# One level of a blocked linear attention summed with tokens as rows, and a two-part activation moved between engines

## The reference

```python
f = 1.0 / (1.0 + np.exp(-f_logit))
for t in range(S):
    state = f[:, :, t, :, None] * state + np.einsum('bhd,bhe->bhde', k[:, :, t], v[:, :, t])
    y[:, :, t] = np.einsum('bhd,bhde->bhe', q[:, :, t], state)
# y as (3072, 384), then
h = x @ w_in                                   # 384 -> 2048
g = np.where(h >= 1, h, np.where(h <= -1, 0.0, (h + 1) ** 2 / 4))
x = g @ w_out                                  # 2048 -> 384
g = x @ w_gate                                 # 384 -> 1536
out = (g * sigmoid(g) * (x @ w_val)) @ w2_out  # 1536 -> 384
```

## Time and profile before the change

| what | value |
|---|---|
| median of three runs | 1029.41 us |
| profiled execution | 1029.71 us, its span 1027.9 us |
| PE busy | 995.3 us, 97% of the span |
| DVE, ACT, POOL busy | 490.3, 466.0, 428.5 us |
| share of PE in the chain that ended last | 89% |
| DMA | 63.61 MB; packets of the SP queue took 16.7% of 16 engines' span |

### The profile page before, as it was taken

How to read it: one execution, slowest core, us unless ns; L and a number is a source line. 1 busy time by engine, 2 the same in 40 slices (tenths; PEclk the granted TensorE clock), 3 DMA queues, 4 the chain that set the end, 5 groups by cost and what they waited for, 6 DMA issues and landing times.

```text
span 1027.9 us, 19928 instructions
## 1 busy us (share of the span) xinstructions
PE 995.3 (97%) x8277; PEld 829.4 (81%) x8277; DVE 490.3 (48%) x615; ACT 466.0 (45%) x851; POOL 428.5 (42%) x360
## 2 busy tenths in 40 slices
PE   4789999999999999999999999999999999999998
PEld 4678688888888888888888888888888888888886
DVE  6879848745954874594355422222222222232221
ACT  5854767657666765766355322221222222221221
POOL 7769736652763565375265222222222222222222
PEclk9989999999999999999999999999999999999999
DMA  9360134015004201300541010010100100000000
GB/s 357 124 226 2 63 99 160 1 44 185 33 2 173 86 2 46 121 32 2 185 139 47 1 62 1 6 56 1 55 7 1 62 1 1 32 0 1 31 1 32
DMA packets 17802, 63.61 MB, mean 62 GB/s; under 512 B 1968, under 2 KB 2352, under 8 KB 16944
## 3 DMA queue, kind: packets, MB, share of 16 engines
q1 hardware_dynamic: 17712, 62.33, 16.7%
HBM read 52.89 MB, written 9.44 MB: 61 GB/s over the span
## 4 chain that ended last, share of the span: by engine, by line
PE 89%; POOL 3%; issue 3%; DVE 2%; ACT 1%; DMA 1%; SPq 0%; ACTq 0%; POOLq 0%; DVEq 0%
PE acc L568 11%; PE acc L569 10%; PE acc L570 10%; PE bank L595 7%; PE bank L594 7%; PE bank L596 7%; PE hid L554 6%; PE hid L556 6%; PE hid L555 6%; PE bank L407 4%; PE hid L595 2%; PE hid L594 2%; PE hid L596 2%; PE bank L474 2%; POOL keys L1120 1%
## 5 line engine op out<-in xcount | busy, mean ns | idle before, releaser
L1162 POOL TENSOR_TENSOR g_lo<-prod,g_hi 128x512 fp32r<-128x512 f32 x72 | 93.1, 1293 | 347.7 <-ACT g_hi L846 347.7
L1155 POOL TENSOR_TENSOR g_lo<-act_tmp,g_hi 128x512 fp32r<-128x512 f32 x96 | 128.2, 1335 | 166.5 <-ACT g_hi L807 166.5
L1053 DVE TENSOR_TENSOR sig<-sig,bank 128x512 f32<-128x512 f32 x72 | 49.6, 688 | 275.4 <-ACT sig L840 275.4
L846 ACT CAST g_hi<-prod 128x512 fp32r<-128x512 f32 x72 | 44.7, 621 | 248.1 <-PE acc L570 248.1
L1120 POOL TENSOR_TENSOR keys<-keys,gates 128x512 f32<-128x512 f32 x82 | 108.1, 1319 | 71.2 <-PE bank L407 46.5
L554 PE MATMUL hid<-x_hi,win_hi 128*128 128x512 f32 (+1 forms) x291 | 116.5, 400 | 0.8 <-DVE act_tmp L1041 0.6
L568 PE MATMUL acc<-g_hi,wout_hi 128*128 128x512 f32 x288 | 114.1, 396 | 1.2 <-POOL g_lo L1155 1.2
L556 PE MATMUL hid<-x_hi,win_lo 128*128 128x512 f32 (+1 forms) x291 | 113.0, 388 | 0.0
L555 PE MATMUL hid<-x_lo,win_hi 128*128 128x512 f32 (+1 forms) x291 | 112.9, 388 | 0.0
L569 PE MATMUL acc<-g_lo,wout_hi 128*128 128x512 f32 x288 | 112.2, 390 | 0.0
L570 PE MATMUL acc<-g_hi,wout_lo 128*128 128x512 f32 x288 | 112.2, 390 | 0.0
(11 more groups left out here) (102 smaller groups left out, 1936.0 us busy)
## 6 DMA issues: line engine op xcount, KB each, us to landing
gates<-in_f_dram SPq DMA_DIRECT2D x12, 512.0 KB, 4.9
queries<-in_q_dram SPq DMA_DIRECT2D x12, 512.0 KB, 4.6
keys<-in_k_dram SPq DMA_DIRECT2D x12, 512.0 KB, 4.7
values<-in_v_tok_dram SPq DMA_DIRECT2D x6, 1024.0 KB, 7.7
q_tok<-in_q_tok_dram SPq DMA_DIRECT2D x12, 384.0 KB, 7.7
k_tok<-in_k_tok_dram SPq DMA_DIRECT2D x12, 384.0 KB, 8.2
x_dram<-x_out SPq DMA_DIRECT2D x6, 768.0 KB, 3.4
x_raw<-x_dram SPq DMA_DIRECT2D x6, 768.0 KB, 5.6
```

What stands on the lines that cost most here:

```text
L1155: pool.tensor_tensor(g_lo[:, c % RING, :], act_tmp[:, 2 + c % 2, :], g_hi[:, c % RING, :].bitcast(F32), ALU.subtract).then_inc(g_lo_done, 1)
```

## The change

Three things change.

1. From the third unit on (`APART = 2`) level 1 is no longer done by PE. The score of a token with the one before it is the sum over 48 dimensions of query times gate times the earlier key. The host lays out gates and queries shifted by one token, with tokens as rows (`f_next`, `q_next`). They are loaded into `q_tok` after its own product is summed; ACT takes the sigmoid (`next_gate`), POOL multiplies the keys by it (`next_key`), the shifted queries are loaded into the same place, DVE multiplies (`next_own`) and sums (`next_sum`) into `nexts`, and four masked copies with `nexts` as the source (`place_nexts`) put them where the two level-1 takes had put theirs. The level's `copy_right`, `level` and `take_level` go; its `scale_q` and `scale_k` stay. The four parts of `place_diag` move to other half slots, and levels 2 to 8 come one half slot earlier.
2. In the first unit the own product and sum come before the scaling of level 32, and no longer wait for POOL's keys.
3. The activation: ACT takes max((h+1)/2, 0) (`Relu`) from the bank, then squares it, and one DVE operation takes the minimum with 1 and the maximum with h. The clamp on DVE is gone.

The core of the diff ("..." where lines are left out):

```diff
-FIRST = Plan(own=(), diag=(20, 22), own_v=(21, 23), ...
+FIRST = Plan(own=(), diag=(18, 20), ... own_v=(21, 22), ...
 def usual(levels, whole, last, y, **others):
-    p = Plan(own=(-13, -12), diag=(-11, -10), own_v=(), place=(-9, -8, -6, -4), sigmoid=(-2, -1), gated=(-1, 0),
+    p = Plan(own=(-13, -12), diag=(-11, -10), own_v=(), next_gate=(-9, -8), next_key=(-8, -7), next_own=(-5, -4), next_sum=(-4, -3), next_place=(1, 2, 3, 4),
+             place=(-5, -3, 0, 1), sigmoid=(-2, -1), gated=(-1, 0),
...
-USUAL = usual((2, 5, 8, 11, 13), 16, 19, 21)
+USUAL = usual((1, 4, 7, 10, 13), 16, 19, 21, sigmoid=(-3, -2), gated=(-2, 0))
+USUAL = USUAL._replace(scale=[0, 1] + USUAL.scale[2:], turn=[0, 1] + USUAL.turn[2:])
...
+        def load_next_gates(a):
+            for g in range(2):
+                sp.wait_ge(diag_done, 2 * a + g + 1)
+                sp.dma_start(tok_group(q_tok, g), tok_group(fn[a], g)).then_inc(fn_in[g], 16)
+        def load_next_queries(a):
+            for g in range(2):
+                sp.wait_ge(next_keyed, 2 * (a - APART) + g + 1)
+                sp.dma_start(tok_group(q_tok, g), tok_group(qn[a], g)).then_inc(qn_in[g], 16)
...
         def attention(a, h):
             for s in placed(PLANS[a].step, h):
-                level(a, s)
+                if s >= apart(a):
+                    level(a, s)
...
+        def next_gate(a, g):
+            act.wait_ge(fn_in[g], 16 * (a - APART + 1))
+            t = tok_group(q_tok, g)
+            act.activation(t, t, ACT.Sigmoid).then_inc(next_gates, 1)
...
         def square(m, c):
-            act.wait_ge(clamped, chunk1(m, c) + 1)
+            n = chunk1(m, c)
+            act.wait_ge(h_ready, n + 1)
...
-            act.activation(t, t, ACT.Square, bias=0.5, scale=0.5).then_inc(squared, 1)
+            act.activation(t, hid[c % 2][:, :], ACT.Relu, bias=0.5, scale=0.5).then_inc(halved, 1)
+            act.wait_ge(halved, n + 1)
+            act.activation(t, t, ACT.Square).then_inc(squared, 1)
...
         def own_first(g):
             dve.wait_ge(qt_in[g], 16)
             dve.wait_ge(kt_in[g], 16)
-            if g == 0:
-                dve.wait_ge(k_scaled, COPIES)
...
+        def next_own(a, g):
+            dve.wait_ge(qn_in[g], 16 * (a - APART + 1))
+            dve.wait_ge(next_keyed, 2 * (a - APART) + g + 1)
+            t = tok_group(q_tok, g)
+            dve.tensor_tensor(t, t, tok_group(k_tok, g), ALU.mult).then_inc(next_owned, 1)
...
+        def place_nexts(a, g, half):
+            dve.wait_ge(next_done, 2 * (a - APART) + g + 1)
+            dve.wait_ge(diag_placed, B * (a - PLAIN) + 2 * (g + 1))
...
+            last = dve.copy_predicated(o, level_mask(0, half), i.broadcast_to([HALF, BP, HALF // 2, 1]))
...
-        def clamp(m, c):
...
-            dve.tensor_scalar(act_tmp[:, c % 2, :], hid[c % 2][:, :], 1.0, -1.0, ALU.min, ALU.max).then_inc(clamped, 1)
...
-            dve.tensor_tensor(act_tmp[:, 2 + c % 2, :], hid[c % 2][:, :], act_tmp[:, c % 2, :], ALU.max
-                              ).then_inc(activated, 1)
+            dve.scalar_tensor_tensor(act_tmp[:, 2 + c % 2, :], act_tmp[:, c % 2, :], 1.0, hid[c % 2][:, :], ALU.min, ALU.max
+                                     ).then_inc(activated, 1)
...
+        def next_key(a, g):
+            pool.wait_ge(next_gates, 2 * (a - APART) + g + 1)
+            t = tok_group(k_tok, g)
+            pool.tensor_tensor(t, t, tok_group(q_tok, g), ALU.mult).then_inc(next_keyed, 1)
```

More of the change, by code:

```diff
@@ L35 @@
 RING = 2
+APART = 2
 TURNED, A_BANK = 3, 5
@@ L67 @@
 H_FIRST = -13
-Plan = namedtuple("Plan", "own diag own_v place sigmoid gated copy step take block_take scale turn whole whole_take last last_take "
+Plan = namedtuple("Plan", "own diag own_v next_gate next_key next_own next_sum next_place place sigmoid gated copy step take block_take scale turn whole whole_take last last_take "
                           "decay y y_out tk tk_out kv state state_place")
-FIRST = Plan(own=(), diag=(20, 22), own_v=(21, 23), place=(), sigmoid=(-6, -5), gated=(-6, -4),
+FIRST = Plan(own=(), diag=(18, 20), next_gate=(), next_key=(), next_own=(), next_sum=(), next_place=(),
+             own_v=(21, 22), place=(), sigmoid=(-6, -5), gated=(-6, -4),
              copy=(-6, -4, 1, 3, 5, 7, 9, 11, 13, 15, 17, 19), step=(0, 2, 4, 6, 8, 10, 12, 14, 16, 18),
@@ L91 @@
 SECOND = usual((6, 9, 12, 14, 16), 18, 21, 23, own=(9, 11), diag=(17, 18), own_v=(19, 20), place=(), sigmoid=(-2, -1),
-               gated=(-1, 1))
-USUAL = usual((2, 5, 8, 11, 13), 16, 19, 21)
-PLANS = [FIRST, SECOND, USUAL._replace(own=(-11, -10), diag=(-9, -8), place=(-7, -6, -5, -4))] + [USUAL] * (UNITS - 3)
+               gated=(-1, 1), next_gate=(), next_key=(), next_own=(), next_sum=(), next_place=())
+USUAL = usual((1, 4, 7, 10, 13), 16, 19, 21, sigmoid=(-3, -2), gated=(-2, 0))
+USUAL = USUAL._replace(scale=[0, 1] + USUAL.scale[2:], turn=[0, 1] + USUAL.turn[2:])
+PLANS = [FIRST, SECOND, USUAL._replace(own=(-11, -10), diag=(-9, -8), next_gate=(-7, -6), next_key=(-6, -5), next_own=(-4, -3), next_sum=(-3, -2))] + [USUAL] * (UNITS - 3)
 W2_EARLY = 5
@@ L117, in turns, with apart, copied @@
     return now
+def apart(a):
+    return 2 if a >= APART else 0
 def fill(a, i):
-    return a * FILLS + i
+    return a * FILLS + max(i, apart(a)) - sum(apart(b) for b in range(a + 1))
+def copied(a, n):
+    return a * COPIES + n - sum(apart(b) for b in range(a + 1))
 def scaled(a, n):
@@ L210, in build @@
     qt_in, kt_in = ([sem(f"{n}_in{g}") for g in range(2)] for n in ("qt", "kt"))
+    fn_in, qn_in = ([sem(f"{n}_in{g}") for g in range(2)] for n in ("fn", "qn"))
     v_in = sem("v_in")
@@ L335, in _ @@
         for a in range(1, UNITS):
+            if a >= APART:
+                load_next_gates(a)
             load_q(a)
@@ L339, in _ @@
             load_k(a)
+            if a >= APART:
+                load_next_queries(a)
             if a > 1:
@@ L398, in level @@
             free(a, s)
[L399 removed]
+            pe.wait_ge(q_copied, copied(a, s + 1))
             if li:
@@ L759, in attention @@
                 sigmoid(a, g)
+            for g in placed(PLANS[a].next_gate, h):
+                next_gate(a, g)
             for s in placed(PLANS[a].copy, h):
-                copy_right(a, s)
+                if s >= apart(a):
+                    copy_right(a, s)
             for g in placed(PLANS[a].block_take, h):
@@ L939, in scale_q @@
             m = LEVELS[li]
-            if s < COPIES:
-                dve.wait_ge(q_copied, a * COPIES + s + 1)
-            else:
+            if apart(a) <= s < COPIES:
+                dve.wait_ge(q_copied, copied(a, s + 1))
+            elif s >= COPIES:
                 dve.wait_ge(filled, fill(a, Y0))
@@ L1006, in attention @@
                 gated(a, g)
+            for g in placed(PLANS[a].next_own, h):
+                next_own(a, g)
+            for g in placed(PLANS[a].next_sum, h):
+                next_sum(a, g)
             for s in placed(PLANS[a].take, h):
-                take_level(a, s)
+                if s >= apart(a):
+                    take_level(a, s)
+            for i in placed(PLANS[a].next_place, h):
+                place_nexts(a, i // 2, i % 2)
             for s in placed(PLANS[a].scale, h):
@@ L1073, in _ @@
                     activate(*((m, c - 1) if c else (m - 1, FC1 - 1)))
-                clamp(m, c)
                 for a, place in turns(m, 2 * c + 1):
@@ L1132, in attention @@
                     own(a, g)
+                for g in placed(PLANS[a].next_key, h):
+                    next_key(a, g)
             for s in placed(PLANS[a].turn, h):
```

42 lines of the change are left out of this document (29 added, 13 removed).

## The result

The changed kernel takes 1035.31 us (median of 5 runs, 1034.17 to 1037.45); the kernel before, run beside it, takes 1029.88 us (median of 5). The ratio is 1.0056, with a 95% interval of [1.0045, 1.0067]: slower by 0.56%, where I had forecast 1.5% faster. The profiled execution of after took 1035.17 us (span 1033.4) against 1029.71 us.

What follows compares the result with a forecast made beforehand. PE's own list was taken to bound the feed-forward stretch. From 1029.71 us, start -6.0, level -9.0, new waits +1.5 and second unit -1.5 gave -15.0: 1014.7 profiled, 1014.4 median, range 1010.0 to 1022.5.

Steps and rivals of the forecast that it cites:

- The level's own price: Third to sixth units: a level on PE costs 2.24 us, so removing it from four units saves 9.0 us.
- go, and four masked copies with the same mask and size come: DVE in later units: four takes (5.44 us together) replaced by four masked copies at 1.36 us each, no change.
- The walk: ACT followed over half slots -8 to 6 where units join, to find waits of PE; 0.4 us a unit taken.
- New waits, +1.5: Four units with the changed level: 0.4 us of new PE waits in each, 1.5 us in all.
- rival 2: ScalarE saturates at the joint of the units; PE waits over 4.1 us a unit, result slower, 1032.9 us; chance 0.05.
- the limit that I had set for being wrong: The forecast counts as wrong if PE's waits after 151 us pass 4 us.
- Rival 1: PE's saving in the units turns into waits: about 7 of 9.0 us come back, 1020.4 us; chance 0.18.
- The start, -6.0: First unit: own product and sum moved into DVE's idle time bring the keys' last transposes 6.0 us earlier, bounds 3.4 to 7.4.
- Rival 3: The start gives only -3 us, because loads or POOL's weight splits set the pace: 1017.4 us; chance 0.14.
- The second unit, -1.5: Second unit's attention, 66 to 151 us: eleven us of clamps leave DVE, ten come to ACT; -1.5 us, between -3 and +1.
- The activation: Per later unit: ACT's second operation adds 10.1 us, sixteen clamps take 11.0 us off DVE, fused operation taken at 0.69 us.

Runs made afterwards that it cites:

- Thin copies: The changed kernel with each of the sixteen masked copies cut to 2 of 32 columns, other next-token scores left out: 1024.89 us, ratio 0.9943 to the kernel before.
- PSUM copies: The changed kernel with the next-token sums written to a free PSUM bank instead of SBUF, plus two waits: 1026.84 us, ratio 0.9963 to the kernel before.
- activation kernel: The kernel before with only the new activation (Relu and square on ACT, one fused operation on DVE): 1033.48 us, ratio 1.0019 to the kernel before.

## Why the prediction was wrong

The forecast for the profiled execution was 1014.7 us, and it took 1035.17. Of these 20.5 us the four units with the changed level are 13.6 (+6.05 against -9.0 + 1.5), the second unit's attention 5.6 (+4.14 against -1.5) and the start 1.3 (-4.74 against -6.0).

- **The level's own price** was right: the later chunks of the unit are as before, and where VectorE's copies are out of the way (PSUM, thin) the units take 88.72 and 88.35 us, against 89.53 before and the 87.3 of the forecast.
- **The step that failed** is "go, and four masked copies with the same mask and size come", priced at "1.36, no change". They took 1.99. That lay inside the bounds I had written, 0.7 to 2.6 times 1.36, but I carried the term into busy time alone, where 2.5 us on an engine with 33 us to spare means nothing. What costs is the other side: POOL's merges, key products and `g_lo` splits in that stretch go from 1.04 to 1.8, from 1.5 to 2.4 and from 1.3 to 2.2 us, and PE waits for POOL. Thin copies (1.1% of the time before, against the changed kernel) and PSUM copies (0.9%, some 9 us) show it, the second with nothing changed but the memory that the source is in and two waits. The copy that met no POOL work took 1.31 us with its source in SBUF, so it is the company and not the source alone. I had the row that says so, 0.96 to 2.59 us beside POOL, and used it for the start and for a bound on the copies' own time, not for what stands beside them; and the Trainium skill's sentence on the shared SBUF interfaces ("GPSIMD Engine Reference", section 1, "Specifications") I used for the start only. Mask and `nexts` are two SBUF inputs; a take from the bank has one.
- **The walk** failed too: I walked ACT and never POOL, whose `g_lo` is what PE waits for. Its key product and merge were hidden by the level that went. That is 1.0 of the remaining 1.4 us a unit. That they hold up the second chunk is shown (it is 4.08 us with them moved); that the units would be at 87.3 with both repaired is not, since no order that I ran gave it. The other 0.4 us are the first chunk's, where ScalarE's late cast and a slow `g_lo` meet.
- **New waits, +1.5**: measured 3.7 a unit, close to the 4.1 from which rival 2 decides. The sign was right, and so was the limit that I had set for being wrong, 4 us of PE's waits after 151 us: the trace has 11.6. The engine was ScalarE only in the first chunk's 0.4 us; the rest is POOL and VectorE. The new places of the placements cost 1.1 us a unit in the old order. In the new one the one at half slot 0 costs nothing measurable, and the one at -3 is part of the first chunk's 0.4. Rival 1 named the saving turned into waits; the saving and 1.5 us a unit more did. (Its sum is off by half a microsecond: with 7 of 9.0 us back and 1.5 already counted, it is 1019.9.)
- **The start, -6.0**: the first half came as worked out (transposes at 59.89 against 59.6), and is worth 1.6 us alone. Some of that agreement is luck: the lower clock came from 40 to 50 us instead of from 50 to 60, in the activation kernel the clock was full there with the old start and the old wait, and the batches' end of 54.6 should have been 54.3 by its own terms (48.2 and four times 1.53). I had followed POOL's splits up to the keys and not asked what of VectorE's would now run beside them. PE's wait came back at 66.87, 2.19 us instead of 3.42, and the lower clock with it. Rival 3, with -3 and POOL's weight splits as its cause, was the better account.
- **The second unit, -1.5**: measured +4.1 (103.47 against 99.33). Some 2.6 us are its first three chunks, where the start's collision lies. Another 1.6 are its last chunk, 5.70 against 4.08 us, which is 4.9 to 6.7 in all versions with the new level; PE waits 1.46 us for the activation there, and VectorE's list has a gate product and the second sum of the third unit ahead of it. That these cause it is argued from the order, not tested.
- **The activation** costs VectorE and ScalarE what I took, and the rule that I named, relu, max and min on VectorE (the Trainium skill, "ScalarE: Activation LUTs", section "Rules for kernel authors"), came out right for the old order (1.0019), though not at the joint where rival 2 had put the loss, and wrong for the new one, where moving the clamp takes 11 us a unit from the list that is late.

## What to carry to other kernels

When a matmul goes, ask which other engine's work its time had covered, and walk the list of every engine that PE waits for, not only the one to which work is added. Price an instruction with two SBUF inputs on VectorE twice, once for itself and once for what GpSimd does beside it. Then look for a place where GpSimd idles, or put one of its sources into PSUM where a bank is free. Work moved earlier meets other company: look at both engines at its new place, and at what its old place kept apart.

## What the runs showed of the hardware

- The collision works both ways and by operand, not by engine load. A masked copy of 64x512 took 1.335 us on the mean with its source in PSUM beside POOL's work, 1.991 (up to 2.30) with it in SBUF, and 1.31 with it in SBUF while POOL was idle. POOL's merge of gates, 1.04 us in the kernel before, took 1.04 beside the copies from PSUM and 1.82 beside those from SBUF.
- It looks like turns, not like a shared rate. Two copies that began 0.88 and 1.10 us before the end of a POOL operation took 2.06 and 2.30 us, so both ended 1.2 us after it. A copy of a sixteenth of the elements (64x32) took 0.22 us at best and 0.91 to 0.97 when it began during a POOL operation: there nearly all of its time is waiting.
- The granted clock doesn't fall after each long wait. After a wait of 3.42 us at 50.9 it was 0.66 on the mean from 50 to 60 us in the kernel before; in the run of the activation alone, after 3.43 us at the same place, 1.00, by its busy times there:

```profile
50.00:60.00 10.00, 6.38 (x163) 5.77 (x155) 7.34 (x9) 5.01 (x8) 10.00 (x6) 1.00 0.78 265
```

In the changed kernel, after a wait of 2.19 us at 64.7, it was 0.83 from 60 to 70 us. Its 0.69 from 40 to 50 us came behind a wait of 2.04 us that ended at 38.53; the kernel before has the same wait of 2.04 us, ending at 40.02, and 1.00 there. How much of the start's gain is the clock's stays open for that reason.
